# Inputs of the recurrent blocks as two half-partition DMAs on two queues, with other edits around the loop (one Trainium2 core)

## The chip, the core and the metric

The program runs on one core of one Trainium2 chip. The metric is device microseconds of one execution, lower is better. In the traces PE is TensorE's matmuls, PEld its weight loads, DVE VectorE, ACT ScalarE, POOL GpSimd, SP the engine whose queue issues DMAs; SPq is the issue of a DMA on it. "L375" is line 375 of the program that is named.

## The reference, cut to what matters

A gated linear recurrence per head (4 batches, 8 heads, 768 steps, 40 features), then a soft mixture of experts on its output, then a product of two projections:

```
for t in range(768):                                  # per batch and head
    m_new = max(f[t] + m, i[t]); C = exp(f+m-m_new)*C + exp(i-m_new)*outer(v, k); n likewise with k
    y[t] = sigmoid(o_gate[t]) * (C @ q) / max(|n @ q|, 1)
x = y as (3072, 320)
logits = x @ phi; d = softmax over tokens; slots = d.T @ x
slot_out = relu(slots @ w1[e]) @ w2[e]                # 8 experts, 4 slots each
x = softmax(logits over slots) @ slot_out
out = (x @ w_a) * (x @ w_b) @ w_out
```

## The kernel before

Engines are programmed one by one, each with an instruction list written out by hand, and meet only through semaphores (`wait_ge`, `then_inc`). The work before the experts is the recurrence in chunked form. The 32 heads are 8 units (u) of 4 heads, and a unit's 768 steps are 3 blocks of 4 chunks of 64 steps: 24 blocks n = 0 to 23, u = n // 3.

**Start.** DVE scans the gates and makes G (running log decay) and b (log input weight less G), each 32x768. Both are cut into three bf16 parts that sum to the f32 value, side by side in the tile `PT`: G's by ACT (casts) and POOL (subtracts, L469), b's by DVE alone (L655 to L658, cast and subtract in turn). SP writes the parts to DRAM (`scratch_b`, `scratch_G`) and `load_exponents(u)` reads each unit's rows back into `LE` and `RE`, the operands of the exponent matmuls. DVE then makes `dm`, from which PE makes the chunk decays, and PE runs 16 transposes that nobody reads (`keep_clock`) before block 0.

**Loop.** In iteration n PE runs `updates(n)`, `exponents(n + 1)`, `scores(n + 1)`, `inner(n)`, `carried(n)` and, from n = 6, `turn(n - 6)`: four transposes (L1026) of finished output, which ACT copies out of PSUM (L545). ACT takes the exponential of `exponents(n)` (L555), POOL scales block n's k by its last column (L491, semaphore `ks_sb`), DVE multiplies scores and exponentials (L684), steps the state (L701) and sums the two output parts (`gather`, L713 and L714); after each unit come a denominator, POOL's product with it (`gate`) and the product with the recurrence's output (`x_out`, L727). The sigmoids of the output gates are ACT's, one batch at a time (L531); the last batch's stands between the exponentials of blocks 1 and 2.

**Loads.** `load_block(n)` on SP is five DMAs: one of k in two layouts on 128 partitions (L375, `kkb`, three buffers), two of q on 40 partitions each (L380) and two of v on 64 each (L386; four buffers each). It waits until the buffer's last readers are done. Behind blocks 8 and 14 SP issues one expert weight tile each (L427, 128x5120 floats), and after the loop two more (L433).

**End.** The last unit isn't finished as a whole: `x_last(n)` on DVE (L735 to L741) finishes blocks 21, 22 and 23 each by itself. `turn(17)` ends iteration 23; `turn(18)` to `turn(23)` follow, through three PSUM banks, all copied by ACT. Then come the logits (first matmuls `ps<-xTreg,small`), the experts and the output tiles, which the change doesn't touch except for the form of two weight loads.

Of the kernel before, what the change touches and what calls it, by code (L numbers as in the profile page):

```python
# [36 lines left out]
ALU = mybir.AluOpType  # L37
# [10 lines left out]
L = 64  # L48
NC = S // L
NCP = NC // 2  # L50
HU = 4
# [58 lines left out]
def build(nc, qT, kk, v1, og, ig, fg, phi, w1, w2, wab, wo, cst, out):  # L110
    with ExitStack() as ctx:
# [63 lines left out]
        qb = [view(take(4 * CB * L), 4 * CB * L).rearrange("r (p h t) -> r p h t", p=2, h=2) for _ in range(NQ)]  # L175

        KF, KT = 2 * CB * L, 2 * HU * D
        kkb = [view(take(KF + KT), KF + KT) for _ in range(3)]
        kb = [x[:, 0:KF].rearrange("r (p t) -> r p t", p=2) for x in kkb]
        knb = [x[:, KF:KF + KT].rearrange("r (c h e) -> r c h e", c=2, h=HU) for x in kkb]  # L180
        VB = 2 * HU * VW + 8
        vb = [view(take(2 * VB), 2 * VB).rearrange("r (a n) -> r a n", a=2) for _ in range(NQ)]
# [3 lines left out]
        Wb = [view(take(512), 512).rearrange("r (c h t) -> r c h t", c=2, h=HU) for _ in range(2)]  # L186
# [10 lines left out]
        def gview(i, n):  # L197
# [65 lines left out]
        ld_k = [sem(f"ld_k{i}") for i in range(3)]  # L263
        ld_q = [sem(f"ld_q{i}") for i in range(NQ)]
        ld_v = [sem(f"ld_v{i}") for i in range(NQ)]
# [98 lines left out]
        def _(sp):  # L364
# [4 lines left out]
            def load_block(n):  # L369
                u, blk = n // NBLK, n % NBLK  # L370
                t0, tn = blk * CB * L, CB * L
                if n >= 3:
                    sp.wait_ge(s_ps, n - 2)
                    sp.wait_ge(ks_sb, n - 2)
                sp.dma_start(kkb[n % 3], kk[u, blk]).then_inc(ld_k[n % 3], 16)  # L375
                if n >= NQ:
                    sp.wait_ge(x_ps, n - NQ + 1)
                for hp in range(2):
                    rows = slice(64 * hp, 64 * hp + D)
                    sp.dma_start(qb[n % NQ][rows, :, hp, :], qT[u, hp, :, :, t0:t0 + tn]).then_inc(ld_q[n % NQ], 16)  # L380
                if n >= NQ:
                    sp.wait_ge(u_ps, n - NQ + 1)
                    sp.wait_ge(y_ps, n - NQ + 1)
                for par in range(2):

                    sp.dma_start(vb[n % NQ][64 * par:64 * par + 64, par, 0:2 * HU * VW],  # L386
                                 v1[u, 64 * par:64 * par + 64, blk, :]).then_inc(ld_v[n % NQ], 16)

            def load_exponents(u):
# [3 lines left out]
                if u == 0:  # L393
                    sp.wait_ge(rows_done, 1)
                    sp.wait_ge(b_out, 16)
                elif u == 1:
                    sp.wait_ge(rows_done_1, 1)
                sp.dma_start(LE[r][L:L + 3 * HU, :], scr_b[u * HU:(u + 1) * HU].rearrange("h k s -> (h k) s")).then_inc(ld_exp[r], 16)
                if u == 0:
                    sp.wait_ge(G_out, 16)  # L400
                for par in range(2):
                    rows = slice(L + R_B + 3 * par, L + R_B + 3 * par + 3)
                    src = scr_G[:, u * HU:(u + 1) * HU].rearrange("k h (c a t) -> k h c a t", a=2, t=L)
                    sp.dma_start(RE[r][rows], src[:, :, :, par, :]).then_inc(ld_exp[r], 16)  # L404

            for b in range(B - 1):
                sp.dma_start(xtok[:, b], og[b]).then_inc(ld_og[b], 16)
            sp.wait_ge(zeroed, 4)
            load_block(0)
# [12 lines left out]
            for n in range(4, NB):
# [3 lines left out]
                if n in (8, 14):  # L426
                    sp.dma_start(w1s[n // 12], w1[n // 12]).then_inc(ld_w1p[n // 12], 16)  # L427
# [4 lines left out]
            for i in (2, 3):  # L432
                sp.dma_start(w1s[i], w1[i]).then_inc(ld_w1p[i], 16)  # L433
# [21 lines left out]
        def _(pool):  # L455
# [11 lines left out]
            for k in range(2):  # L467
                pool.wait_ge(cut_done, k + 1)
# [55 lines left out]
        def _(act):  # L524
# [14 lines left out]
            for b in range(B - 1):  # L539
                sigmoid(b)  # L540
# [772 lines left out]
```

## Time and profile before

| | |
|---|---|
| median of 3 runs | 290.74 us (290.41 to 292.62) |
| profiled execution, its own time | 292.25 us |
| its span, first to last instruction | 290.2 us |
| mean granted TensorE clock | 0.965 of full |
| busy: PE, PEld, DVE, ACT, POOL | 250.7, 208.8, 181.8, 88.3, 61.8 us |
| loop (block 0's exponents to the end of `turn(17)`) | 23.0 to 142.9 us |
| first logits | 147.35 us |

Rows are from the profiled execution, in us from the span's start. A timeline row is: start, duration, engine, line, operation, output<-input, shapes, count, and in brackets how long the engine had been idle before it and who ended that.

### The profile page before, as it was taken

The numbers are of one execution on the slowest core, as the hardware profiler recorded it, in microseconds if no ns is written. First come the engines' busy times: TensorE is split into PE (matmuls) and PEld (weight loads), VectorE is DVE, ScalarE is ACT, GpSimd is POOL, SyncE is SP. The second block draws the span as 40 slices with busy tenths as digits, with TensorE's granted clock in tenths as the row PEclk, the third lists the DMA queues.
The fourth block names the chain that finished last, engine by engine and source line by source line (L and its number), as shares of the span: only waits on it lengthen the run. The fifth ranks groups of instructions, "written<-read, shape, count | busy, mean of one in ns | idle before, by whom it ended". The sixth has DMA issues, their size and how long they took to land.

```text
span 290.2 us, 7910 instructions
## 1 busy us (share of the span) xinstructions
PE 250.7 (86%) x3264; PEld 208.8 (72%) x3264; DVE 181.8 (63%) x462; ACT 88.3 (30%) x145; POOL 61.8 (21%) x92
## 2 busy tenths in 40 slices
PE   0557698855999499999799998999799999999996
PEld 0546687845999499899657935556656668999995
DVE  6963667842787277888916823355886867555550
ACT  3683511210222113222236002343800003444441
POOL 9502152311325123427030321331000000000000
PEclk9999999995899779999999999999979999999999
DMA  7827866689658965660299999990000000322222
GB/s 247 351 52 252 221 189 196 183 370 262 179 149 323 288 190 153 184 203 2 78 420 419 424 416 381 436 399 24 2 0 0 0 2 0 113 93 90 80 82 90
DMA packets 20131, 54.73 MB, mean 189 GB/s; under 512 B 3744, under 2 KB 14144, under 8 KB 18432
## 3 DMA queue, kind: packets, MB, share of 16 engines
q1 hardware_dynamic: 20096, 54.23, 54.1%
q8 instruction: 26, 0.43, 0.6%
q14 instruction: 9, 0.07, 0.1%
HBM read 49.99 MB, written 4.23 MB: 187 GB/s over the span
## 4 chain that ended last, share of the span: by engine, by line
PE 60%; SPq 12%; DVE 11%; DMA 11%; issue 2%; ACT 2%; DVEq 0%
PE ps L935 52%; DMA attn<-kk 8%; SPq L380 5%; SPq L386 4%; PE ps L1148 3%; PE ps L1026 2%; DVE attn L701 1%; SPq L375 1%; ACT xTreg L545 1%; DMA attn<-scratch_G 1%; DMA scratch_G<-xTreg 1%; PE ps L1154 1%; DMA xTreg<-ig 1%; SPq L404 1%; DVE attn L684 1%
## 5 line engine op out<-in xcount | busy, mean ns | idle before, releaser
L935 PE MATMUL ps<-attn 128*64 128x41 f32 (+3 forms) x2016 | 92.4, 253 | 17.9 <-DMA attn<-kk 10.4
L935 PEld LDWEIGHTS ps<-attn 128*64 128x64 f32 (+1 forms) x2016 | 86.7, 141 | 25.1 <-DMA attn<-kk 10.9
L491 POOL TENSOR_TENSOR attn<-attn 128x160 f32<-128x160 f32 x48 | 21.1, 461 | 86.2 <-issue 54.4
L701 DVE SCALAR_TENSOR_TENSOR attn<-attn,small,ps 128x41 f32<-128x41 f32 x176 | 31.0, 249 | 5.0 <-PE ps L935 5.0
L545 ACT COPY xTreg<-ps 128x512 f32<-128x512 f32 x24 | 13.6, 593 | 63.8 <-PE ps L1026 63.8
L935 PE MATMUL ps<-woreg,tlow 128*128 128x320 f32 x96 | 28.0, 454 | 2.5 <-DVE tlow L885 2.5
L935 PE MATMUL ps<-Whr,Phr 128*128 128x320 f32 x96 | 30.0, 313 | 0.0
L935 PE MATMUL ps<-Whr,Plr 128*128 128x320 f32 x96 | 29.7, 309 | 0.0
L935 PE MATMUL ps<-Wlr,Phr 128*128 128x320 f32 x96 | 29.6, 309 | 0.0
L684 DVE TENSOR_TENSOR attn<-ps,attn 128x512 f32<-128x512 f32 x24 | 16.5, 688 | 19.6 <-issue 13.6
L935 PEld LDWEIGHTS ps<-woreg,tlow 128*128 128x128 f32 x96 | 18.4, 200 | 11.8 <-DVE tlow L885 4.6
L555 ACT ACTIVATE attn<-ps 128x512 f32<-128x512 f32 x24 | 14.3, 597 | 27.3 <-PE ps L935 27.3
L904 DVE TENSOR_TENSOR Plr<-tail,Phr 128x512 fp32r<-128x512 f32 x20 | 13.8, 691 | 13.0 <-ACT Phr L610 13.0
L713 DVE TENSOR_TENSOR attn<-ps,small 128x328 f32<-128x328 f32 x24 | 12.0, 498 | 14.1 <-PE ps L935 14.1
L935 PEld LDWEIGHTS ps<-Whr,Phr 128*128 128x128 f32 x96 | 18.0, 188 | 0.6 <-issue 0.5
L935 PEld LDWEIGHTS ps<-Wlr,Phr 128*128 128x128 f32 x96 | 18.0, 188 | 0.1
L935 PEld LDWEIGHTS ps<-Whr,Plr 128*128 128x128 f32 x96 | 18.0, 188 | 0.0
L587 ACT COPY tail<-ps 128x512 f32<-128x512 f32 x20 | 10.8, 589 | 18.5 <-PE ps L1148 18.5
L318 POOL TENSOR_TENSOR freg<-small 128x512 f32<-128x512 f32 x6 | 8.6, 1429 | 34.6 <-PE ps L1148 22.0
L318 DVE TENSOR_TENSOR freg<-small 128x512 f32<-128x512 f32 x18 | 12.5, 718 | 5.4 <-PE ps L1148 5.4
L1026 PE MATMUL ps<-small,xreg 128*80 128x128 f32 x96 | 14.9, 287 | 0.8 <-ACT xTreg L545 0.8
L610 ACT CAST Phr<-tail 128x512 fp32r<-128x512 f32 x20 | 12.1, 620 | 10.7 <-PE ps L935 10.7
(158 smaller groups left out, 339.8 us busy)
## 6 DMA issues: line engine op xcount, KB each, us to landing
attn<-kk SPq DMA_DIRECT2D x24, 416.0 KB, 4.5
front<-w SPq DMA_DIRECT2D x2, 2560.0 KB, 10.6
tail<-w SPq DMA_DIRECT2D x2, 2560.0 KB, 12.1
xTreg<-w SPq DMA_DIRECT2D x4, 1280.0 KB, 12.9
attn<-v SPq DMA_DIRECT2D x48, 82.0 KB, 3.2
xreg<-og SPq DMA_DIRECT2D x4, 960.0 KB, 7.0
attn<-qT SPq DMA_DIRECT2D x48, 80.0 KB
xreg<-w SPq DMA_DIRECT2D x3, 1280.0 KB, 10.9
```

The source lines that it names most:

```text
L318: return eng.tensor_tensor(Pt[t % 4], fixed(Ed[:, t], 16), shifted(Ed[:, t], 0, 16), ALU.mult)
L380: sp.dma_start(qb[n % NQ][rows, :, hp, :], qT[u, hp, :, :, t0:t0 + tn]).then_inc(ld_q[n % NQ], 16)
L491: last = g.tensor_tensor(ksb[n % 2][:, c, 0:HU * D].rearrange("r (h e) -> r h e", h=HU), knb[n % 3][:, c], last_col[:, c].unsqueeze(2).to_ ...
L545: s.copy(xT[:, u % 2, u // 2, CB * blk:CB * blk + CB].rearrange("r c t -> r (c t)"), turn_ps(m)[:, :]).then_inc(xT_sb, 1)
L555: s.activation(Eb[n % 2], psE[n % 2][:], ACT.Exp).then_inc(e_sb, 1)
L610: s.copy(Ph[t % 3], Pm[t]).then_inc(one["ph_sb"], 1)
L684: v.tensor_tensor(Wb[n % 2].rearrange("r c h t -> r (c h t)"), psS[n % 2][:], Eb[n % 2], ALU.mult).then_inc(w_sb, 1)
L701: last = v.scalar_tensor_tensor(out=C[:, cc + 1, p], in0=C[:, cc, p], scalar=dcy[:, 2 * u + p, cc:cc + 1], in1=pUv[:, p, c, 0:VW], op0=ALU ...
L713: chain(v.tensor_tensor(T, pXv[:, :, :, 0:VW], eg.unsqueeze(3).to_broadcast([128, 2, CB, VW]), ALU.mult))
L904: v.tensor_tensor(Pl[t % 3], Pm[t], Ph[t % 3].bitcast(F32), ALU.subtract).then_inc(one["pl_sb"], 1)
L935: return t_.matmul(o_, l_, r_, start=start, stop=stop)
L1026: last = t_.transpose(turn_ps(m)[0:80, 128 * c:128 * c + 128], xtok[:, u // 2, blk * CB + c, 80 * (u % 2):80 * (u % 2) + 80], ident)
```

## The change

1. **Blocks by halves.** q, v and k of a block lie in one DRAM array and one tile `in_b` (four buffers, 2512 columns). Partitions 0 to 63 take columns 0 to 1671, partitions 64 to 127 columns 840 to 2511; q is padded from 40 to 64 rows. SP loads the lower half, ACT's queue the upper one (`load_upper`; in the loop after the exponential of block n - 2). All of a block's readers wait for both halves, and both wait for all readers of the buffer four blocks ago.
2. **Parts of b** by four two-input subtracts; the casts are gone (L710 to L714 of the program after).
3. **First unit's operands** go from `PT` to `LE` and `RE` straight, by 10 small DMAs; the DRAM copies serve units 1 to 7. G's parts are stored with the even and the odd chunks apart, so a read of them is 768 bytes in a row (128 before).
4. **Gates** by tanh: sigmoid(x) = 0.5 tanh(x/2) + 0.5, two ACT instructions for half a batch, spread over the loop. The list that is built has one table load for all of ACT's start and loop; before it had five.
5. **Weights in pieces.** w1's first two tiles come as 10 pieces of 128x1024 behind blocks 4 to 15, except 6 and 12, where a batch of gates is loaded; the last two tiles as 10 pieces after the loop.
6. **End.** DVE keeps the denominators (`den_last`) and block 23's products; POOL takes those of 21 and 22. `turn(17)` stands ahead of `carried(23)`; DVE copies `turn(21)` and `turn(23)` out of PSUM, ACT the rest.
7. DVE's product of scores and exponentials goes to another tile (`Ed`'s place in `small`).

```diff
+        in_b = [view(take(HALF + OTHER), HALF + OTHER) for _ in range(NQ)]
+        qb = [two(x, 0, [[CB * L, 2], [HALF + VF, 2], [1, CB * L]]) for x in in_b]
+        vb = [two(x, QF, [[VF + KF + KT, 2], [1, VF + 8]]) for x in in_b]
@@ SP
             def load_block(n):
-                sp.dma_start(kkb[n % 3], kk[u, blk]).then_inc(ld_k[n % 3], 16)
-                for hp in range(2):
-                    sp.dma_start(qb[n % NQ][rows, :, hp, :], qT[u, hp, :, :, t0:t0 + tn]).then_inc(ld_q[n % NQ], 16)
-                for par in range(2):
-                    sp.dma_start(vb[n % NQ][64 * par:64 * par + 64, par, 0:2 * HU * VW],
-                                 v1[u, 64 * par:64 * par + 64, blk, :]).then_inc(ld_v[n % NQ], 16)
+                if n >= NQ:
+                    done = n - NQ + 1
+                    sp.wait_ge(s_ps, done)
+                    sp.wait_ge(ks_sb, done)
+                    sp.wait_ge(u_ps, done)
+                    sp.wait_ge(y_ps, done)
+                    sp.wait_ge(x_ps, done)
+                else:
+                    sp.wait_ge(zeroed, n + 1)
+                sp.dma_start(in_b[n % NQ][0:64, 0:HALF], blk_in[u, blk, 0]).then_inc(ld_b[n % NQ], 16)
...
             sp.wait_ge(parts_b, 1)
+            for h in range(HU):
+                sp.dma_start(LE[0][L + 3 * h:L + 3 * h + 3, :], PT[h:h + 1, :, S:2 * S]).then_inc(ld_exp[0], 16)
+            sp.wait_ge(parts_G, 1)
+            for par in range(2):
+                for k in range(3):
+                    row = L + R_B + 3 * par + k
+                    sp.dma_start(RE[0][row:row + 1].rearrange("r h c t -> r h (c t)"), PT[0:HU, k, 384 * par:384 * par + 384]).then_inc(ld_exp[0], 16)
...
-                if n in (8, 14):
-                    sp.dma_start(w1s[n // 12], w1[n // 12]).then_inc(ld_w1p[n // 12], 16)
+                if n in (6, 12):
+                    sp.dma_start(xtok[:, n // 6 + 1], og[n // 6 + 1]).then_inc(ld_og[n // 6 + 1], 16)
+                elif 4 <= n < 16:
+                    j = n - 4 - (n > 6) - (n > 12)
+                    cols = slice(j % 5 * F, j % 5 * F + F)
+                    sp.dma_start(w1s[j // 5][:, cols], w1[j // 5, :, cols]).then_inc(ld_w1p[j // 5], 16)
@@ ACT
+            for n in range(3):
+                load_upper(n)
             act.wait_ge(ld_const, 16)
...
+            def sigmoid(u):
+                act.wait_ge(ld_og[u // 2], 16)
+                x = xtok[:, u // 2, :, 80 * (u % 2):80 * (u % 2) + 80]
+                s.activation(x, x, ACT.Tanh, scale=0.5).then_inc(tanh_done, 1)
+                act.wait_ge(tanh_done, u + 1)
+                s.activation(x, x, ACT.Copy, scale=0.5, bias=0.5).then_inc(sig_done, 1)
...
             for n in range(NB):
-                if n == 2:
-                    sigmoid(B - 1)
...
                 s.activation(Eb[n % 2], psE[n % 2][:], ACT.Exp).then_inc(e_sb, 1)
+                if 2 <= n < NB - 2:
+                    load_upper(n + 2)
+                if n >= 4 and n % NBLK == 1 and n // NBLK + 1 < NU:
+                    sigmoid(n // NBLK + 1)
                 if n >= 7:
                     xT_evac(n - 7)
@@ DVE
             chain(v.tensor_tensor(b_, t2_g, GB[:, 0:S], ALU.subtract))
-            chain(v.tensor_copy(PT[:, 0, S:2 * S], b_))
+            chain(v.tensor_tensor(PT[:, 0, S:2 * S], t2_g, GB[:, 0:S], ALU.subtract))
             chain(v.tensor_tensor(R, b_, PT[:, 0, S:2 * S], ALU.subtract))
-            chain(v.tensor_copy(PT[:, 1, S:2 * S], R))
+            chain(v.tensor_tensor(PT[:, 1, S:2 * S], b_, PT[:, 0, S:2 * S], ALU.subtract))
@@ PE
                 inner(n)
+                if n == NB - 1:
+                    turn(n - 6)
                 carried(n)
```

The order at three places. **First place, SP's queue from the load of block 8 to that of block 9** (`kk`, `qT`, `v`: the five DMAs of a block; `w`: expert weights). Before:

```order
L375 DMA attn<-kk 128x832 [waits ks_sb,s_ps]
L380 DMA attn<-qT 40x2x256 [waits x_ps]
L380 DMA attn<-qT 40x2x256
L386 DMA attn<-v 64x328 [waits y_ps,u_ps]
L386 DMA attn<-v 64x328
L427 DMA front<-w 128x5120
L375 DMA attn<-kk 128x832 [waits ks_sb,s_ps]
```

After, from behind block 6 to behind block 8 (`blk_in`: a block's lower half; `og`: gates):

```order
L444 DMA xreg<-og 128x1920
L404 DMA attn<-blk_in 64x1672 [waits y_ps,u_ps,x_ps,ks_sb,s_ps]
L414 DMA attn<-scratch_b 12x768 [waits e_ps]
L418 DMA attn<-scratch_G 3x4x384 x2
L448 DMA front<-w 128x1024
L404 DMA attn<-blk_in 64x1672 [waits y_ps,u_ps,x_ps,ks_sb,s_ps]
L448 DMA front<-w 128x1024
```

Between two blocks stands now at most a fifth of a weight tile, or a batch of gates.

**Second place, the start.** ACT before, from its first row to G's second part:

```order
L334 ACT_TABLE_LOAD
L334 CAST attn<-small 82x768 [waits ld_const]
L337 CAST attn<-small 76x384 x4
L535 CAST xTreg<-xTreg 32x768 [waits G_done]
L536 ACTIVATE xTreg<-xTreg 32x768
L538 CAST xTreg<-xTreg 32x768 [waits R_done]
```

ACT after, the same stretch (`zeroed`: POOL has cleared the buffer):

```order
L574 DMA attn<-blk_in 64x1672 [waits zeroed] x3
L339 ACT_TABLE_LOAD
L339 CAST attn<-small 82x768 [waits ld_const]
L342 CAST attn<-small 76x384 x4
L590 CAST xTreg<-xTreg 32x6x2x64 [waits G_done]
L591 ACTIVATE xTreg<-xTreg 32x768
L593 CAST xTreg<-xTreg 32x6x2x64 [waits R_done]
L574 DMA attn<-blk_in 64x1672 [waits zeroed]
```

Three half loads, which wait for POOL's clears, stand now ahead of ACT's table load and of all that it does for G.

**Third place, DVE's end of the loop**, from the scores of block 23 to its own products. Before:

```order
L684 TENSOR_TENSOR attn<-ps,attn 128x512 [waits y_ps,s_ps,e_sb]
L735 SCALAR_TENSOR_TENSOR attn<-attn 128x2x4 [waits t_sb]
L736 TENSOR_SCALAR attn<-attn 128x2x4 [waits dve]
L738 TENSOR_TENSOR xreg<-xreg,attn 128x2x4x40 [waits sig_done,dve]
L740 RECIPROCAL attn<-attn 128x2x4
L741 TENSOR_TENSOR xreg<-xreg,attn 128x2x4x40 [waits dve]
L713 TENSOR_TENSOR attn<-ps,small 128x2x164 [waits x_ps,y_ps]
L714 TENSOR_TENSOR attn<-attn,ps 128x2x164 [waits dve]
```

After, the same stretch:

```order
L740 TENSOR_TENSOR small<-ps,attn 128x512 [waits y_ps,s_ps,e_sb]
L789 SCALAR_TENSOR_TENSOR attn<-attn 128x2x4 [waits t_sb]
L790 TENSOR_SCALAR attn<-attn 128x2x4 [waits dve]
L791 RECIPROCAL attn<-attn 128x2x4 [waits dve]
L769 TENSOR_TENSOR attn<-ps,small 128x2x164 [waits x_ps,y_ps]
L770 TENSOR_TENSOR attn<-attn,ps 128x2x164 [waits dve]
```

The two products of block 21 are gone from DVE's list ahead of block 22's `gather`; those of block 22 are gone in the same way ahead of block 23's.

## Rows read from the trace of the kernel before

**Rows 1.** The page, the chain that ended last, by engine.

```profile
PE 60%; SPq 12%; DVE 11%; DMA 11%; issue 2%; ACT 2%; DVEq 0%
```

**Rows 2.** Timeline of PE, turns and what stands between them.

```profile
55.98 0.63 PE L1026 MATMUL ps<-small,xreg 128*80 128x128 f32 x4
...
60.04 0.64 PE L1026 MATMUL ps<-small,xreg 128*80 128x128 f32 x4
...
68.42 4.92 PE L935 MATMUL ps<-attn 128*64 128x128 f32 x64 [6.71 <-DMA attn<-kk]
73.27 1.04 PE L1026 MATMUL ps<-small,xreg 128*80 128x128 f32 x4
...
94.35 0.63 PE L1026 MATMUL ps<-small,xreg 128*80 128x128 f32 x4
...
104.55 0.77 PE L1026 MATMUL ps<-small,xreg 128*80 128x128 f32 x4
```

**Rows 3.** Windows: busy us (instructions) by engine, then clock, DMA share, GB/s.

```profile
117.04:129.59 12.55, 12.39 (x267) 11.48 (x265) 10.31 (x36) 3.55 (x6) 4.54 (x8) 1.00 0.71 196
170.00:190.00 20.00, 19.12 (x196) 10.31 (x186) 6.58 (x11) 6.25 (x12) 4.88 (x3) 1.00 1.00 414
```

**Rows 4.** The chain in order of time, 55 to 70 us: start, us, what.

```profile
56.96 11.42 DMA attn<-kk
```

**Rows 5.** DMA issues by line, ns min/median/max, and landings.

```profile
L386 SPq DMA_DIRECT2D attn<-v x48: 529/590/1762, 9.0 to 128.3; - x48
...
DMA to landing us min/median/max: 2.3/3.2/9.6
```

**Rows 6.** DMA in 104 to 131 us: packets, MB, share of 16 engines.

```profile
q1 hardware_dynamic: 3173, 4.59, 60.6%
...
attn<-kk SPq DMA_DIRECT2D x5, 416.0 KB, 3.8
```

**Rows 7.** Timeline of the start, DVE and POOL.

```profile
9.79 0.94 DVE L654 TENSOR_TENSOR xTreg<-xTreg 32x768 f32<-32x768 f32 x1
9.92 2.31 POOL L469 TENSOR_TENSOR xTreg<-xTreg 32x768 f32<-32x768 f32 x1 [2.80 <-ACT xTreg L535]
10.77 1.88 DVE L655 CAST xTreg<-xTreg 32x768 bf16<-32x768 f32 x1
...
13.17 1.95 POOL L469 TENSOR_TENSOR xTreg<-xTreg 32x768 bf16<-32x768 f32 x1 [0.94 <-ACT xTreg L538]
13.66 1.88 DVE L657 CAST xTreg<-xTreg 32x768 bf16<-32x768 f32 x1
15.57 0.94 DVE L658 TENSOR_TENSOR xTreg<-xTreg 32x768 bf16<-32x768 f32 x1
16.45 0.54 DVE L334 CAST attn<-small 82x768 bf16<-82x768 f32 x1
```

**Rows 8.** Timeline, a POOL and a DVE product of the experts' stage.

```profile
196.64 1.15 POOL L318 TENSOR_TENSOR freg<-small 128x512 f32<-128x512 f32 x1 [5.03 <-PE ps L1148]
...
197.03 1.31 DVE L318 TENSOR_TENSOR freg<-small 128x512 f32<-128x512 f32 x1 [0.50 <-PE ps L1148]
```

**Rows 9.** Timeline of PE and ACT, first iterations.

```profile
19.45 3.65 PE L1032 MATMUL ps<-small 128*128 128x128 f32 x16
...
25.20 2.43 PE L935 MATMUL ps<-attn 128*64 128x128 f32 x48 [0.67 <-DMA attn<-qT]
...
29.51 1.80 ACT L531 ACTIVATE xreg<-xreg 128x1920 f32<-128x1920 f32 x1 [3.03 <-DMA xreg<-og]
...
32.00 3.36 PE L935 MATMUL ps<-attn 128*64 128x128 f32 x80 [1.47 <-issue]
...
36.20 1.07 PE L935 MATMUL ps<-attn 82*64 82x256 bf16 x16 [0.85 <-DMA attn<-scratch_G]
```

**Rows 10.** Timeline of ACT and PE, end of the loop.

```profile
144.26 3.04 ACT L545 COPY xTreg<-ps 128x512 f32<-128x512 f32 x6 [0.79 <-PE ps L1026]
...
147.35 3.11 PE L935 MATMUL ps<-xTreg,small 128*32 128x384 f32 x36
```

More of the change, by code:

```diff
@@ L107, in constants, with build @@
     return c
-def build(nc, qT, kk, v1, og, ig, fg, phi, w1, w2, wab, wo, cst, out):
+def build(nc, blk_in, og, ig, fg, phi, w1, w2, wab, wo, cst, out):
     with ExitStack() as ctx:
@@ L185, in build @@
               for _ in range(2)]
-        Wb = [view(take(512), 512).rearrange("r (c h t) -> r c h t", c=2, h=HU) for _ in range(2)]
+        Wb = [Ed[:, 8 * i:8 * i + 8].rearrange("r (c h) t -> r c h t", c=2) for i in range(2)]
         Eb = [view(take(512), 512) for _ in range(2)]
@@ L262, in build @@
         ld_w2e = [sem(f"ld_w2e{i}") for i in range(E)]
-        ld_k = [sem(f"ld_k{i}") for i in range(3)]
-        ld_q = [sem(f"ld_q{i}") for i in range(NQ)]
-        ld_v = [sem(f"ld_v{i}") for i in range(NQ)]
+        ld_b = [sem(f"ld_b{i}") for i in range(NQ)]
         ld_exp = [sem(f"ld_exp{i}") for i in range(2)]
@@ L401, in load_exponents @@
                 for par in range(2):
                     rows = slice(L + R_B + 3 * par, L + R_B + 3 * par + 3)
[L403 to L409, printed above, removed]
-            sp.wait_ge(parts_b, 1)
+                    src = scr_G[:, u * HU:(u + 1) * HU].rearrange("k h (a s) -> k h a s", a=2)
@@ L432, in _ @@
             for i in (2, 3):
-                sp.dma_start(w1s[i], w1[i]).then_inc(ld_w1p[i], 16)
+                for j in range(5):
+                    cols = slice(j * F, j * F + F)
+                    sp.dma_start(w1s[i][:, cols], w1[i, :, cols]).then_inc(ld_w1p[i], 16)
             sp.wait_ge(one["logits_ps"], 2)
@@ L465, in _ @@
             pool.wait_ge(C_zero, 2)
-            for k in range(2):
-                pool.wait_ge(cut_done, k + 1)
-                left = g.tensor_tensor([GR, PT[:, 2]][k][:, 0:S], [GB, GR][k][:, 0:S], PT[:, k, 0:S], ALU.subtract)
-                left.then_inc([R_done, parts_G][k], 1)
+            pool.wait_ge(cut_done, 1)
+            g.tensor_tensor(by_par(GR[:, 0:S]), by_par(GB[:, 0:S]), halves(0), ALU.subtract).then_inc(R_done, 1)
+            pool.wait_ge(cut_done, 2)
+            g.tensor_tensor(halves(2), by_par(GR[:, 0:S]), halves(1), ALU.subtract).then_inc(parts_G, 1)
             pool.wait_ge(parts_G, 1)
@@ L503, in _ @@
                         last.then_inc(x_sb, 1)
+            for i in range(2):
+                T, d, x = last_unit(NB - NBLK + i)
+                pool.wait_ge(den_done, NU + i)
+                pool.wait_ge(sig_done, NU)
+                for p in range(2):
+                    last = g.tensor_tensor(x[:, p], x[:, p], T[:, p, :, 0:D], ALU.mult)
+                last.then_inc(last_half, 1)
+                pool.wait_ge(last_half, i + 1)
+                for p in range(2):
+                    last = g.tensor_tensor(x[:, p], x[:, p], d[:, 1, p].unsqueeze(2).to_broadcast([128, CB, D]), ALU.mult)
+                last.then_inc(last_sb, 1)
             pool.wait_ge(y_ps, NB)
@@ L756, in _ @@
             gather(NB - 1)
+            den_last(NB - 1)
             x_last(NB - 1)
+            for m in (NB - 3, NB - 1):
+                v_.wait_ge(t_ps, m + 1)
+                v.tensor_copy(turned(m), turn_ps(m)[:, :]).then_inc(xT_sv, 1)
             v.memset(ones, 1.0)
```

155 lines of the change are left out of this document (81 added, 74 removed).

## The prediction

> **What bounds the kernel now.** I read the chain that ended last first: 60% of it is PE, but 12% is SP's issuing and 11% DMA [rows 1], so PE isn't bound by its own work everywhere. The timeline of PE shows where. One `turn` ends each iteration of the loop, so the distance of two turns is an iteration. At 55.98 and 60.04 they are 4.06 us apart; the next is at 73.27, because PE stood idle for 6.71 us for k of the next block and then ran 64 matmuls in 4.92 us [rows 2]. The chain names the transfer: k was issued at 56.96 and took 11.42 us, as it was queued behind the 2.6 MB weight tile [rows 4]. The same again between 94.35 and 104.55 [rows 2]. Undisturbed, three iterations take 12.55 us with PE busy in 12.39 of them [rows 3]: 4.18 each, PE-bound, and no edit touches PE's work there. After the loop the experts' stage is PE's (19.12 of 20 us busy, while the DMA engines run full at 414 GB/s [rows 3]), and the change leaves its order alone. So there are four places to cost: the two stalls, the transfers that replace them, the start, and the end of the loop.
>
> **The two stalls.** They cost 73.27 - 60.04 - 4.06 = 9.17 and 104.55 - 94.35 - 4.06 = 6.14 us, 15.3 in all, the slow matmuls behind them included [rows 2]. In pieces, a block waits for at most 0.52 MB (1.27 us at 414 GB/s) or a batch of gates of 0.98 MB (2.37 us), where an undisturbed k took 3.8 us from issue to landing [rows 6]. **-15.3**, if nothing else in the DMA queue is late next.
>
> **What is late next: the DMA engines.** A block is now 128 x 1672 x 4 bytes = 0.856 MB (0.758 before). What rate do half-partition transfers reach? In 104 to 131 us, where only blocks were loaded, 4.59 MB took 60.6% of 27 us: 281 GB/s per busy time [rows 6]. That is a mix. The five k transfers (2.13 MB, 128 partitions) at 414 would take 5.1 of the 16.4 busy us; the other 2.46 MB, all on 64 partitions or fewer, then ran at 2.46 / 11.3 = 217. So the bounds are 217 and 414 GB/s. I take 281: half a partition range, but long rows (6.7 KB), and two queues whose halves can lie over each other.
> The time that is available, from the load of block 4 (0.6 us into iteration 1) to `scores(15)` (1.0 into iteration 14): five iterations without a turn at 3.8 (below), eight at 4.18, and 0.4 more, less 2.0 for landing (2.3 at least for an 82 KB transfer [rows 5], 0.3 of it its bytes) = 50.8 us. Needed: 12 blocks x 3.05 = 36.6, 9 pieces x 1.27 = 11.4, 2 batches of gates x 2.37 = 4.7, together 52.7. Short by 1.9; I add 1.2 because a load can't run further ahead than four buffers, so that the two batches come as bursts. **+3.1** as short waits in iterations 6 to 13. At 414 GB/s it is 0, at 217 it is 12 x 3.94 + 16.1 - 50.8 + 1.2 = 13.8. From block 16 on 3.05 is under 4.18 and hidden. A load's wait for all readers of the buffer adds nothing: before, q and v waited for the same block, and the operands and the piece that stand behind it on SP are due iterations later.
>
> **ACT's new work.** An upper half's issue is not in the trace; SP's for 64 partitions takes 0.59 us [rows 5]. ACT is busy for 3.55 / 3 = 1.18 us of an iteration [rows 3]; with the issue 1.8, and with the tanh and the copy (half of 1.80 each [rows 9]) 3.6 in every third one. The next exponential is due 3.8 to 4.2 us after the last, so this is hidden; `load_upper`'s waits (block n - 2 done) have passed before the exponential of block n can start. It would cost once an issue took over 1 us.
>
> **The start** has three terms.
> *Parts of b, +0.9.* Before, two casts of 1.88 and two subtracts of 0.94 ended at 16.51 [rows 7]. But a wider cast takes 0.54 [rows 7]: the two ended 0.4 us after POOL's subtracts did (12.23 and 15.12), and POOL's own first one (9.92) lay over DVE's subtract to 10.73. Each waits for the other, and a DVE product with two SBUF inputs does so too: 1.31 us for 128x512 when a POOL product ran until 197.79 [rows 8]. Replacing the casts therefore doesn't save 2 x 0.94. Four subtracts end at 10.77 + 4 x 0.98 = 14.7 if POOL never holds them; with both of POOL's (12.23 - 10.73 = 1.5 each) in between, at 17.7. ACT's part comes later as well: three half loads wait for POOL's clears ahead of it. I take 17.2, that is +0.7. Block 0's exponents follow 6.5 us behind by PE (decays and the 16 transposes of 3.65 us up to 23.1 [rows 9]), or by SP: ten issues of 0.3 to 0.6 and a landing of 2.3 or more, 5.3 to 8.5 us. Say +0.9 in all; ends -1.8 and +3.
> *First iterations, -3.0.* PE's waits for q (0.67), for q and k behind the gates' batch (1.47) and for unit 1's operands (0.85) go [rows 9]: blocks 0 to 2 are loaded long before, and with the tanh there is no table load or sigmoid (29.51 [rows 9]) between the exponentials of blocks 1 and 2. Unit 1's operands are issued at about 26 and due at 33.
> *Iterations 2 to 6, -1.6.* From 36.20 [rows 9] to 55.98 [rows 2] is 19.8 us. An iteration without a turn needs 4.18 less the turn's 0.6 on PE, and DVE some more: 3.8 (3.6 at the least). From the exponents to an iteration's end is 3.0, so 3.0 + 4 x 3.8 = 18.2. SP's five issues per block become one.
> Together **-3.7** (ends -7 and 0).
>
> **The end, -1.3.** Two pairs of products (0.49 us each) leave DVE ahead of the last two `gather`s, which PE and then everything wait for. After it ACT copied six turns in 3.04 us, right up to the logits [rows 10]; now DVE takes two, and `turn(17)` fills an idle stretch of PE. DVE's chain then ends about 1 us earlier and the last copies 0.3 sooner behind it; 0 if POOL, which takes those products in four operations of 0.45 us, is late.
>
> **The sum.** -15.3 + 3.1 - 3.7 - 1.3 = -17.2 us. Against the profiled execution's own 292.25 this is 275.0; that execution lay 1.5 above the median of the runs, so against 290.74 it is **273.5 us**. The experts' stage moves as a whole: its weights are asked for at the loop's end as before, and ten issues of 0.6 us instead of two stay behind transfers of 1.27.
>
> **Rivals.** *Fast transfers.* The two halves overlap fully, 320 GB/s or more: no short waits, 270.4; with parts of b that POOL doesn't hold (-2.5), 267.9. For it: rows of 6.7 KB. Chance 0.18.
> *The halves take turns.* Transfers to partitions 0 to 63 and 64 to 127 run one after the other at half width, 217 GB/s as above [rows 6]: +13.8 instead of +3.1, 284.2. For it: that rate is what the half-wide transfers of this trace give. Against it: those were short and shared one queue. Chance 0.12.
> By the Trainium skill, page "SBUF — State Buffer", section "Can I just issue two DMAs to hit both halves?", two such DMAs side by side ran only 6% faster than one, and its table has 196 GB/s for one of 1 MiB on partitions 0 to 63. By that rule a block takes 0.856 / 208 = 4.1 us and the kernel about 286, an estimate; this trace, which has no pair of long halves, shows neither.
> *Slower than before.* The same mechanism with a lower rate. The whole gain of 20.3 us (without transfers' cost) is gone when 12 t + 16.1 - 50.8 + 1.2 + 8 (t - 4.18) = 20.3, t being a block's transfer: t = 4.35 us, 197 GB/s. At 180 GB/s t is 4.76 and the kernel takes 298.6: PE would wait for `blk_in` in every iteration to the last. Against it: no stretch of block loads in the trace is that slow per busy time. Chance 0.04.
>
> **How the numbers follow.** The likeliest, 0.66: 270 to 278. The range 268 to 282 leaves out most of the turn-taking rival and the slower one, and some of the fastest. A measurement of this kernel tells changes over about 1% from none. Faster by over 1%, under 287.8: all but the slower case and a little of the turn-taking one, 0.94; within 1% 0.03; slower 0.03.
>
> **What the profile after will show.** Turns 4.1 to 4.5 us apart with no idle of several us and a granted clock of 1.00 throughout; short PE waits for `blk_in` in iterations 6 to 13, and 0.9 DMA share there; DVE's subtract chain with one or two of 1.5 to 2.5 us and an end near 17; block 0's exponents near 24; `turn(17)` near 124; logits about 17 us earlier than 147.35. It is wrong if the turns drift to 5 us (rate of halves), if ACT's issues take over 1 us, or if the start lies 3 us off.

## The result, and the profile after

The changed kernel takes **302.71 us** (median of 4 runs, 302.33 to 304.38), the kernel before beside it 290.69 (290.41 to 292.62): 1.041 times as long, 95% interval 1.035 to 1.047. The forecast was 273.5, with 282 as its upper end. The profiled execution has a span of 300.7 us against 290.2. The profiled execution of the kernel before took 292.25 us, 1.5 more than its median, so a difference between traces comes out that much more favourable to a change. Some kernels below have executions that took over 1.5% longer than their fastest one; where a reading hangs on them, all times are given.

The chain that ended last now names the blocks' loads. Before, issues of SP held 12% of it and DMA 11% [rows 1]; now SP's issuing is 2%, and DMA 18%, nearly all of it one tensor:

```profile
PE 62%; DMA 18%; DVE 12%; issue 3%; SPq 2%; ACT 1%; ACTq 0%; DVEq 0%
PE ps L997 53%; DMA attn<-blk_in 17%; PE ps L1212 3%; PE ps L1087 2%; DVE attn L757 2%; SPq L432 1%; SPq L427 1%; DVE xTreg L713 1%; DVE xTreg L711 1%; PE ps L1093 1%; PE ps L1218 1%; DMA xTreg<-ig 1%; DVE attn L769 1%; ACT freg L622 1%; DV
```

PE's timeline has lost the two big stalls of [rows 2], and has gained many smaller ones. The first turn comes at 63.62 instead of 55.98, the next ones lie 5.5 to 8.1 us apart, and only from 121.34 on is the distance 4.06 again:

```profile
63.62 0.78 PE L1087 MATMUL ps<-small,xreg 128*80 128x128 f32 x4
...
67.58 1.98 PE L997 MATMUL ps<-attn 128*64 128x128 f32 x16 [2.14 <-DMA attn<-blk_in]
...
71.71 0.63 PE L1087 MATMUL ps<-small,xreg 128*80 128x128 f32 x4
...
77.90 1.08 PE L1087 MATMUL ps<-small,xreg 128*80 128x128 f32 x4
...
121.34 0.63 PE L1087 MATMUL ps<-small,xreg 128*80 128x128 f32 x4
125.40 0.63 PE L1087 MATMUL ps<-small,xreg 128*80 128x128 f32 x4
```

The windows say why (busy us by engine, then granted clock, DMA share, GB/s). Over 90 us the DMA engines are fully busy and move 227 to 249 GB/s. The experts' stage, again at share 1.0, moves 420 (414 in [rows 3]). So a share of 1.0 isn't a rate; the two columns have to be read together. PE's clock is granted at 0.83 on the mean of 45 to 75 us, a mixture of its two levels (1.2 and 2.4 GHz); PE stands idle for 7.8 of these 30 us, nearly all of it in waits for blocks:

```profile
30.00:45.00 15.00, 12.65 (x304) 11.73 (x302) 11.80 (x45) 4.40 (x6) 4.53 (x8) 1.00 1.00 249
45.00:75.00 30.00, 22.20 (x386) 20.75 (x388) 13.95 (x46) 5.57 (x8) 6.25 (x12) 0.83 1.02 227
75.00:120.00 45.00, 32.81 (x636) 28.68 (x631) 26.09 (x86) 14.31 (x20) 11.55 (x21) 0.96 1.02 234
...
162.00:182.00 20.00, 19.34 (x216) 15.09 (x212) 12.95 (x33) 5.22 (x10) 3.81 (x2) 1.00 1.02 420
```

The DMA view of the same 90 us (30 to 120) has the queues (q1 is SP's, q10 ACT's: packets, MB, share of the 16 engines' time) and what was queued: count, size, and median time from issue to landing. A half takes some 12 us to land (5 where only blocks are loaded); pieces and gates, which are 128 partitions wide, are later still:

```profile
q1 hardware_dynamic: 3455, 14.70, 72.0%
q10 hardware_dynamic: 1148, 6.16, 28.8%
...
attn<-blk_in SPq DMA_DIRECT2D x15, 418.0 KB, 11.9
attn<-blk_in ACTq DMA_DIRECT2D x15, 418.0 KB, 12.6
front<-w SPq DMA_DIRECT2D x10, 512.0 KB, 17.5
xreg<-og SPq DMA_DIRECT2D x2, 960.0 KB, 18.1
```

In 121 to 146 us only blocks are loaded, as in the window of [rows 6]: (2.29 + 2.19) MB in 74.1% of 25 us is 242 GB/s per busy time.

```profile
q10 hardware_dynamic: 432, 2.29, 38.2%
q1 hardware_dynamic: 459, 2.19, 35.9%
```

At the start, each of DVE's rounding subtracts ends 0.8 us after POOL's beside it (13.06 and 12.24, 16.35 and 15.54), which is nearly the 0.94 us that one takes undisturbed: it seems to start its work only when POOL's has ended. Below are DVE and POOL, then SP's issues of the ten small transfers, then PE:

```profile
10.44 1.80 POOL L491 TENSOR_TENSOR xTreg<-xTreg 32x768 f32<-32x768 f32 x1 [3.42 <-ACT xTreg L590]
10.79 2.27 DVE L711 TENSOR_TENSOR xTreg<-xTreg 32x768 bf16<-32x768 f32 x1
...
13.19 2.35 POOL L493 TENSOR_TENSOR xTreg<-xTreg 32x768 bf16<-32x768 f32 x1 [0.94 <-ACT xTreg L593]
14.07 2.28 DVE L713 TENSOR_TENSOR xTreg<-xTreg 32x768 bf16<-32x768 f32 x1
16.39 0.94 DVE L714 TENSOR_TENSOR xTreg<-xTreg 32x768 bf16<-32x768 f32 x1
```

```profile
17.43 2.96 SPq L427 DMA_DIRECT2D attn<-xTreg  x4
20.43 3.74 SPq L432 DMA_DIRECT2D attn<-xTreg  x6
```

```profile
25.28 3.04 PE L997 MATMUL ps<-attn 82*64 82x256 bf16 x56 [1.74 <-DMA attn<-xTreg]
```

### The profile page after: what moved, and what is told of

It is laid out like the page before. It is cut to its first block, busy times and chain, and to the rows that moved or that the text cites. A ratio compares the mean times of both kernels' runs of the same rounds, so it can differ in the third digit from the quotient of the medians.

```text
span 300.7 us, 7912 instructions
## 1 busy us (share of the span) xinstructions
PE 252.1 (84%) x3264; PEld 209.4 (70%) x3264; DVE 183.2 (61%) x460; ACT 91.2 (30%) x151; POOL 65.2 (22%) x100
## 3 DMA queue, kind: packets, MB, share of 16 engines
q10 hardware_dynamic: 1920, 10.27, 14.2%
## 4 chain that ended last, share of the span: by engine, by line
PE 62%; DMA 18%; DVE 12%; issue 3%; SPq 2%; ACT 1%; ACTq 0%; DVEq 0%
PE ps L997 53%; DMA attn<-blk_in 17%; PE ps L1212 3%; PE ps L1087 2%; DVE attn L757 2%; SPq L432 1%; SPq L427 1%; DVE xTreg L713 1%; DVE xTreg L711 1%; PE ps L1093 1%; PE ps L1218 1%; DMA xTreg<-ig 1%; DVE attn L769 1%; ACT freg L622 1%; DVE tlow L384 1%
## 5 line engine op out<-in xcount | busy, mean ns | idle before, releaser
L997 PE MATMUL ps<-attn 128*64 128x41 f32 (+3 forms) x1632 | 80.5, 255 | 26.1 <-DMA attn<-blk_in 17.2
L997 PEld LDWEIGHTS ps<-attn 128*64 128x64 f32 (+1 forms) x1632 | 70.6, 142 | 34.5 <-DMA attn<-blk_in 19.9
L514 POOL TENSOR_TENSOR attn<-attn 128x160 f32<-128x160 f32 x48 | 21.1, 460 | 98.2 <-DMA attn<-blk_in 46.7
L740 DVE TENSOR_TENSOR small<-ps,attn 128x512 f32<-128x512 f32 x24 | 16.6, 691 | 23.4 <-issue 16.5
L600 ACT COPY xTreg<-ps 128x512 f32<-128x512 f32 x22 | 12.7, 587 | 57.2 <-PE ps L1087 57.2
L997 PE MATMUL ps<-woreg,tlow 128*128 128x320 f32 x96 | 26.8, 437 | 2.7 <-DVE tlow L947 2.7
L997 PEld LDWEIGHTS ps<-woreg,tlow 128*128 128x128 f32 x96 | 17.4, 190 | 11.9 <-DVE tlow L947 5.3
L997 PE MATMUL ps<-attn,small 128*64 128x96 f32 x384 | 22.3, 259 | 0.0
L997 PEld LDWEIGHTS ps<-attn,small 128*64 128x64 f32 x384 | 19.8, 145 | 0.2
```

Source lines behind the costliest of these rows:

```text
L514: last = g.tensor_tensor(ksb[n % 2][:, c, 0:HU * D].rearrange("r (h e) -> r h e", h=HU), knb[n % NQ][:, c], last_col[:, c].unsqueeze(2).to ...
L600: s.copy(turned(m), turn_ps(m)[:, :]).then_inc(xT_sb, 1)
L740: v.tensor_tensor(Wb[n % 2].rearrange("r c h t -> r (c h t)"), psS[n % 2][:], Eb[n % 2], ALU.mult).then_inc(w_sb, 1)
L997: return t_.matmul(o_, l_, r_, start=start, stop=stop)
```

## The experiments

I ran twelve kernels in three groups, each group against the kernel before on the same chip: 289.81 us (288.81 to 291.73) for e1 to e4, 289.27 (287.88 to 291.19) for e5 to e8, 289.98 (288.76 to 291.37) for e9 to e12. A ratio is to that; intervals are of 95%. The first group was run when only the trace above was known: the halves, the two queues, the pieces and the total of bytes were all suspects.

**e1, both halves in one queue.**

```diff
+                sp.dma_start(in_b[n % NQ][64:128, OTHER:OTHER + HALF], blk_in[u, blk, 1])...
-                s.dma_start(in_b[n % NQ][64:128, OTHER:OTHER + HALF], ...)   # ACT's, in load_upper
```

> The kernel after, with both halves of a block issued on SP, one behind the other (ACT issues none). Three theories of why the loop's DMA engines moved only 234 GB/s. Half width: a transfer into 64 partitions reaches about half the rate wherever it is issued: stays slow, 298 to 308 us, 200 to 240 GB/s at a share of 1.0 in the loop. Two queues: the two queues' packets disturb each other and one queue would not: 276 to 285 us. Bytes: the rate belongs to the mix of reads and no form helps: 300 to 305 us.

Measured: 309.40 us, ratio 1.068 (1.061 to 1.075), just over the 298 to 308 of the half-width theory. The four runs are 305.30, 308.04, 310.76 and 310.94; even the fastest is above the changed kernel's slowest, 304.38. Its window 45 to 75, at the same share as above:

```profile
45.00:75.00 30.00, 20.33 (x406) 18.32 (x404) 15.95 (x55) 6.15 (x10) 7.36 (x14) 0.93 1.02 232
```

One queue isn't better than two: by the two faster runs it is 1 to 2% worse, by the median 2.6%. So two queues were not what slowed the kernel. By the Trainium skill, page "SBUF — State Buffer", section "Can I just issue two DMAs to hit both halves?", two such transfers side by side gain only 6% over one; the traces agree in kind (from 30 to 120 us the loop moves 234 GB/s with two queues and 230 with one).

**e2, whole blocks of full width.** The host writes the zeros that the two halves leave out, so a block is one transfer of 128 x 2512 numbers: 1.286 MB instead of 0.856.

```diff
-                sp.dma_start(in_b[n % NQ][0:64, 0:HALF], blk_in[u, blk, 0])...
+                sp.dma_start(in_b[n % NQ], blk_in[u, blk])...
-                s.dma_start(in_b[n % NQ][64:128, OTHER:OTHER + HALF], ...)   # ACT's
```

> The kernel after, each block as ONE transfer of the whole tile, 128 partitions x 2512 columns (1.286 MB, zeros included, 50% more bytes) on SP. Half width: 1.286 / 414 = 3.1 us per block instead of about 3.8, the loop needs 12 x 3.1 + 16.1 = 53 us for 51 available, so stalls of at most 5 us in all: 275 to 283 us. Two queues: the same, as there is one queue. Bytes: 234 GB/s stays, 5.5 us per block: over 320 us.

Measured: **280.74 us**, ratio 0.969 (0.963 to 0.975). With half as many bytes again per block, the kernel takes 22 us less than the changed one. Window 45 to 75:

```profile
45.00:75.00 30.00, 27.31 (x584) 24.53 (x582) 22.86 (x77) 10.16 (x15) 9.80 (x18) 1.00 1.01 412
```

The same engines at the same share move 412 GB/s where the halves move 227. PE waits for `blk_in` for 1.7 us in all instead of 17.2.

**e3, k at full width, q and v by halves.** 128 x 832 in one transfer, and 64 x 840 in each queue.

```diff
+                sp.dma_start(in_b[n % NQ][:, OTHER:HALF], kk_in[u, blk])...
+                sp.dma_start(in_b[n % NQ][0:64, 0:OTHER], blk_in[u, blk, 0])...
+                s.dma_start(in_b[n % NQ][64:128, HALF:HALF + OTHER], blk_in[..., 1])...
```

> The kernel after, k of a block as one 128-partition transfer of 832 columns on SP, q and v as two halves of 64 x 840, on SP and ACT as before. Bytes as in the kernel after. Half width: 0.43 MB at 414 and 0.43 at about 235, 2.9 us per block: 276 to 286 us. Two queues: both queues still at work, so 290 to 303 us. Bytes: 300 to 305 us.

Measured: 291.78 us, ratio 1.005 (1.001 to 1.009), between e2 and the changed kernel at the changed kernel's bytes. Half of a block's bytes at full width give 269 GB/s in 45 to 75 us, at share 1.04. This is a miss: the half-width theory had said 276 to 286, and 290 to 303 was what disturbance between two queues would give. By itself e3 speaks for the queues; e6 below decides against them.

**e4, the pieces alone, in the kernel before.**

```diff
-                if n in (8, 14):
-                    sp.dma_start(w1s[n // 12], w1[n // 12])...
+                if 4 <= n < 16 and n not in (6, 12):
+                    sp.dma_start(w1s[j // 5][:, cols], w1[j // 5, :, cols])...
```

> The kernel before with one edit alone: the first two weight tiles in ten pieces of 128x1024 behind blocks 4 to 15 (not 6 and 12). Blocks keep their five transfers. If the price of the change is in the block transfers, the two stalls of 9.2 and 6.1 us go and little comes in their place: 275 to 280 us. If the pieces themselves (their 4 KB rows among the blocks) are what slowed the loop: 290 to 300 us.

Measured: 283.86 us, ratio 0.979 (0.974 to 0.983), less of a gain than expected. From the first turn to the logits it takes 78.6 us instead of 91.4, so most of the two stalls is gone. But the first turn comes at 61.53 instead of 55.98: in iterations 3 to 6 PE now stands idle, 3.03 us at one place. The row gives that wait no releaser, but the chain that ended last names k of block 6: SP issues it at 45.24, right behind a piece (44.56), and it lands 6.46 us later, where an undisturbed k takes 3.8 [rows 6]. POOL waits 4.71 us for it, and PE goes on 1.33 us after it has landed. How much of the 6.46 is the piece's is not separated.

```profile
53.03 6.66 PE L937 MATMUL ps<-attn 128*64 128x128 f32 x116 [3.03 <-issue]
```

e2 differs from the changed kernel in width, row length, bytes and ACT's issues all at once. The second group takes them apart. In e5 and e6 half of the partitions don't get the columns that the computation needs, so the two stand for the time alone.

**e5, the same bytes at full width.** Each block one transfer of 128 x 1672.

```diff
-                sp.dma_start(in_b[n % NQ], blk_in[u, blk])...              # e2
+                sp.dma_start(in_b[n % NQ][:, 0:HALF], blk_in[u, blk])...
```

> The changed kernel with every block loaded by one transfer of 128 partitions x 1672 numbers on SP's queue: the 0.856 MB of the two halves, at full width (e2 moved 1.286 MB a block). The columns of q, v and k then stand wrong for partitions 64 to 127 and the last 840 columns stay as cleared, so this run computes other numbers; its instructions and times are otherwise those of the changed kernel. Theory A (half the partitions make the rate): the blocks run at 400 GB/s or more, 2.1 us each, no wait of PE for a block after iteration 2, 272 to 279 us, at or some us below e2's 280.7. Theory B (the row length of 6.7 KB, and its mixture with pieces of 1.3 to 4 KB rows, makes the rate): 235 GB/s as in the changed kernel, about 300 us.

Measured: **276.15 us**, ratio 0.954 (0.947 to 0.961). Bytes, row length (6.7 KB) and pieces are those of the changed kernel; only the width isn't, and there is one queue. Beside e1, which has one queue too, a block is one transfer of 128 x 1672 instead of two of 64 x 1672: 276.15 us against 309.40. The DMA view of 30 to 120 us, against the one above:

```profile
q1 hardware_dynamic: 5216, 25.55, 78.0%
...
attn<-blk_in SPq DMA_DIRECT2D x20, 836.0 KB, 6.5
front<-w SPq DMA_DIRECT2D x10, 512.0 KB, 7.5
xreg<-og SPq DMA_DIRECT2D x2, 960.0 KB, 9.2
```

That is 25.55 / (0.78 x 90) = 364 GB/s per busy time, less than the 400 that I had expected, and 20.86 / (1.008 x 90) = 230 with the halves. Theory B (row length and mixture) falls.

**e6, the same at full width, by two queues.** Two transfers of 128 x 836, SP's and ACT's.

```diff
+                sp.dma_start(in_b[n % NQ][:, 0:HALF // 2], blk_in[u, blk, 0])...
+                s.dma_start(in_b[n % NQ][:, HALF // 2:HALF], blk_in[..., 1])...   # load_upper
```

> As e5, with the 1672 numbers of each of 128 partitions in two transfers of 836, one on SP's queue and one on ACT's: both queues and ACT's issues as in the changed kernel, the same bytes, full width. It leaves the same part of the computation wrong as e5. Theory A (half width): as e5, 272 to 279 us. Theory C (two queues at once, or ACT's issues in its row): most of the loss is still there, 290 us or more. Shorter rows (3.3 KB) may cost a little: up to 3 us above e5 under theory A.

Measured: **275.09 us**, ratio 0.950 (0.943 to 0.957). It issues from the same engines at the same places as the changed kernel, with the same bytes, at the same semaphores. Theory C falls too. Its window 45 to 75, and its turns, which are undisturbed from first to last (only three of the rows stand here):

```profile
45.00:75.00 30.00, 28.39 (x625) 26.23 (x621) 24.20 (x83) 11.02 (x16) 10.25 (x19) 1.00 0.99 363
```

```profile
55.09 0.63 PE L1087 MATMUL ps<-small,xreg 128*80 128x128 f32 x4
59.15 0.63 PE L1087 MATMUL ps<-small,xreg 128*80 128x128 f32 x4
...
121.88 0.63 PE L1087 MATMUL ps<-small,xreg 128*80 128x128 f32 x4
```

**e7, e2 with the pieces later.**

```diff
-                elif 4 <= n < 16:
+                elif n in (8, 9, 10, 13, 14, 16, 17, 18, 20, 21):
```

> e2 (whole blocks of 1.286 MB at full width) with the ten pieces of w1's first two tiles behind blocks 8, 9, 10, 13, 14, 16, 17, 18, 20 and 21 instead of 4 to 15. If in e2 the DMA engines were what PE waited for in iterations 2 to 10 (their share was near 1 there, PE waits for blocks 1.7 us), this takes 2 to 4 us off: 277 to 279. If they weren't, it is e2's 280.7.

Measured: 279.58 us, ratio 0.965 (0.959 to 0.970). The interval overlaps e2's, so by the times it is unclear. In the traces the way from the first turn to the logits is 134.29 - 56.66 = 77.6 us against 136.19 - 55.62 = 80.6: 3 us shorter, as expected; but the matmuls at the start take 1.5 us longer in this trace (see e9).

**e8, the changed kernel with whole weight tiles.**

```diff
-                elif 4 <= n < 16:
-                    sp.dma_start(w1s[j // 5][:, cols], w1[j // 5, :, cols])...
+                if n in (8, 14):
+                    sp.dma_start(w1s[n // 12], w1[n // 12])...
```

> The changed kernel with w1's first two tiles whole again, behind blocks 8 and 14: only the splitting of the weights is undone. If the loop of the changed kernel is bound by the total of its transfers at some 235 GB/s, as I now think, splitting them hardly matters: 299 to 306 us, the waits gathered at two places of 8 to 12 us. If the pieces themselves are slow or in the blocks' way, this is faster, under 297. If pieces save what I forecast (two stalls of 15.3 us in all), it is slower, 313 or more.

Measured: 302.02 us (296.10, 301.80, 302.23 and 306.79; they spread too far for a ratio), beside the changed kernel's 302.71. This rules out that the pieces save 15 us here, for that needed 313 or more. It doesn't decide between "hardly matters" (299 to 306) and "faster" (under 297), as the fastest run lies in the latter. In the trace, of the slowest run, the lost time is gathered at four places where turns lie 8.9 to 11.5 us apart, and 30 to 120 us move 228 GB/s, as the changed kernel's 234. That fits a loop bound by the total of its transfers, but does not show it.

The third group asks for the small terms, on e7.

**e9, the first unit's operands through memory again.**

```diff
-            for h in range(HU):
-                sp.dma_start(LE[0][...], PT[h:h + 1, :, S:2 * S])...
-            for par in range(2):
-                for k in range(3):
-                    sp.dma_start(RE[0][row:row + 1]..., PT[0:HU, k, ...])...
             sp.dma_start(scr_b, ...); sp.dma_start(scr_G, ...)
+            load_exponents(0)
```

> e7 (whole blocks at full width, pieces later) with the first unit's operands by way of device memory again, as the kernel before has them (three loads in place of ten, behind the two stores). In e7 the ten small transfers keep SP for 6.7 us and PE waits 1.3 us for the last one. Expected: block 0's exponents at 24.0 instead of 25.3, by PE's own transposes, and 1 to 1.5 us less in all: about 278. If the detour through memory costs the 2 us of landing that it was made to save, they stay at 25 or later and the time at 279.6.

Measured: **275.62 us**, ratio 0.950 (0.945 to 0.955), 4 us better than e7 (of the group before) where 1 to 1.5 were expected. PE's rows of e7, of e11 and of e9, in this order:

```profile
25.35 4.56 PE L992 MATMUL ps<-attn 82*64 82x256 bf16 x56 [1.34 <-DMA attn<-xTreg]
```

```profile
25.28 3.05 PE L990 MATMUL ps<-attn 82*64 82x256 bf16 x56 [1.34 <-DMA attn<-xTreg]
```

```profile
23.74 3.08 PE L987 MATMUL ps<-attn 82*64 82x256 bf16 x56
```

The exponents start at 23.74 with no wait, 1.6 us earlier. Another 1.5 us are of a kind that I hadn't expected: the matmuls behind the wait took 4.45 to 5.8 us in the traces of e1, e3, e5, e7, e8 and e10, and 3.05 in those of the changed kernel, e2, e6 and e11, behind the same wait. Without it (e9, e12) they took 3.04 and 3.08. In e9 the detour begins at 17.24 with a store and its last load is issued by 21.1; in e7 the last of the ten direct transfers is issued at 24.2. Of the lead, 3.0 us stand at the exponential of block 4 and 2.3 are left at the logits. Another 1.2 us lie behind them, in the part that the edit doesn't touch; that part takes 141.8 to 143.1 us in the fourteen traces, with no order that an edit explains. So the traces give the direct transfers a price of 2.3 to 3.0 us; for the rest of the 4 they show no cause.

**e10, the casts back.**

```diff
-            chain(v.tensor_tensor(PT[:, 0, S:2 * S], t2_g, GB[:, 0:S], ALU.subtract))
+            chain(v.tensor_copy(PT[:, 0, S:2 * S], b_))
```

and the same for the second part.

> e7 with the two casts back in place of the subtracts that round parts of b. Expected: DVE's chain ends at 16.5 instead of 17.4, the exponents 0.8 us earlier at 24.5, the time about 279, within what a measurement can tell. If the differences save what two casts of 1.88 against two subtracts of 0.94 would (1.9 us), they end at 19 or later and the run is slower by 1.5.

Measured: 279.51 us, ratio 0.963 (0.959 to 0.967): no difference from e7 that the times can show. In the trace parts of b end 1 us sooner and block 0's exponential starts at 24.99 instead of 26.02. At the first turn 0.8 us of it are left, at the logits none (134.34 against 134.29). A cast waits for POOL as the subtract does, but takes 1.88 us there and the subtract 2.28:

```profile
10.63 1.88 DVE L706 CAST xTreg<-xTreg 32x768 bf16<-32x768 f32 x1
...
13.53 1.88 DVE L708 CAST xTreg<-xTreg 32x768 bf16<-32x768 f32 x1
```

**e11, the gates by a sigmoid.**

```diff
-                s.activation(x, x, ACT.Tanh, scale=0.5)...
-                s.activation(x, x, ACT.Copy, scale=0.5, bias=0.5)...
+                s.activation(x, x, ACT.Sigmoid)...
```

> e7 with the gates by one sigmoid in place of a tanh and a copy, still one unit at a time. I forecast that the tanh takes a table load (1.3 us) from between the exponentials and makes iterations 0 to 2 shorter. Expected: a table load before and after each of the eight gates' functions, 2.6 us of ACT each time, two of them before block 0's exponentials (hidden) and six in the loop; ACT is idle for 2.5 us of an iteration, so each costs PE at most 1 us: 280 to 285. If ACT's slack takes them all, 279.6.

Measured: 278.39 us, ratio 0.960 (0.956 to 0.964); the interval overlaps e7's, and the sigmoid is in no case slower. ACT's slack takes both table loads of each unit (ACT's timeline of e11):

```profile
39.54 0.60 ACT L602 ACTIVATE attn<-ps 128x512 f32<-128x512 f32 x1 [3.34 <-PE ps L990]
40.15 1.28 ACT L583 ACT_TABLE_LOAD   x1
41.45 1.00 ACT L583 ACTIVATE xreg<-xreg 128x960 f32<-128x960 f32 x1
42.47 1.28 ACT L602 ACT_TABLE_LOAD   x1
43.83 0.60 ACT L602 ACTIVATE attn<-ps 128x512 f32<-128x512 f32 x1
```

From `turn(0)` to `turn(17)` both e11 and e7 take 71.5 us. The tanh brought nothing, and the 280 to 285 that I had expected without it were too dear.

**e12, e9 and e10 together**: whole blocks at full width, pieces behind later blocks, casts, operands through memory.

> e7 with both the casts and the way through device memory back: e9 and e10 together. Expected: exponents of block 0 at 23.1 as in the kernel before, 2.2 us earlier than in e7, and 277.4 us. If the rest of the loop is bound by its transfers, which start no earlier, less of it arrives: 278.5.

Measured: **274.55 us**, ratio 0.948 (0.943 to 0.953), exponents at 22.51. It is 2.9 us better than expected. By the median this is the fastest of those that do the whole computation, though its interval overlaps e9's: 15.4 us below the kernel before, some 28 below the changed one.

## Why the prediction was wrong

The stretches of the loop, in us of the profiled executions. Exp(n) is ACT's exponential of block n; the forecast is the sum of the prediction's terms for that stretch. By the medians the changed kernel is 12.0 us slower and e6 14.2 faster, where these traces have 10.5 and 17.0: the trace of the kernel before is of an execution of 292.25 us, 1.5 above the median beside the changed kernel and 3.0 above the one beside e6.

| stretch | before | forecast | after | e6 |
|---|---|---|---|---|
| start to Exp(0) | 23.49 | +0.9 | +2.2 | +2.2 |
| Exp(0) to Exp(4) | 16.53 | -3.0 | -3.3 | -2.9 |
| Exp(4) to `turn(0)` | 15.96 | -1.6 | +8.7 | -0.3 |
| `turn(0)` to `turn(16)` | 82.11 | -15.3 + 3.1 | +4.8 | -15.3 |
| `turn(16)` to logits | 9.26 | -1.3 | -0.9 | -0.9 |
| logits to the end | 142.85 | 0 | -1.0 | +0.2 |
| sum | 290.2 | -17.2 | +10.5 | -17.0 |

**The step that failed is "What is late next": "I take 281: half a partition range, but long rows (6.7 KB), and two queues whose halves can lie over each other", with the pieces and gates costed at 414 beside it.** The blocks alone run at 242 GB/s, nearer to the lower bound of 217 than to 281, and the second queue is worth 1 to 2.6% of the time (e1), not a rate between the two bounds. The larger error is the other half of the sum: pieces (512 KB) and gates (960 KB) were costed as if they ran by themselves. They are 128 partitions wide, but share the engines with the halves, and the whole loop moves 230 GB/s. The 17.0 MB of my sum (12 x 0.856 + 9 x 0.524 + 2 x 0.983) then need 74 us of the 50.8, short by 23 and not by 1.9. Of these 21 us more, 6 are the blocks' own rate (12 x 0.856 at 242 instead of 281) and 15 come from the company that they keep. Measured against e6, which has the same bytes at full width, the term was 8.9 + 20.1 = 29 us instead of 3.1. The windows from the exponential of block 4 to `turn(16)` take it apart: both kernels run 1724 matmuls there, the changed one in 88.1 busy us of 111.5 at a mean clock of 0.94, e6 in 79.8 of 82.5 at 1.00. So 20.7 us are idle time of PE and 8.3 are matmuls that ran slower behind the waits, a cost for which the sum had no term. The sign that the prediction had named for this, turns that drift to 5 us, is what the trace shows: 5.5 to 8.1.

**The rivals.** "The halves take turns" was nearest to the mechanism (that width sets the rate is shown, that the two halves literally alternate is not) and "Slower than before" the outcome, with a threshold set too low, at 197 GB/s for the block (196 when its sum is worked out again). That threshold came from a sum with 16.1 us for pieces and gates. With all 17.0 MB at one rate r, the whole gain of 20.3 us is gone when 17.0 / r = 50.8 - 1.2 + 20.3 = 69.9 us, that is at 243 GB/s; the trace's 230 lies just under it. Such a rate was inside the bounds that I had given for the blocks (217 to 414), so with everything in the queue at the blocks' rate "slower" would have been near even, and not a chance of 0.04.

**The two stalls**, -15.3: right, had nothing else been late. In e6 the stretch that held them is 15.3 us shorter, and in e4 the pieces alone give back 12.8 between first turn and logits.

**ACT's new work**: right that it is hidden. An issue takes 0.47 us, and e6, with all of ACT's issues, has turns 4.06 apart. But what I credited the tanh with, in -3.0 for the first iterations, was not its doing: the size was right (-3.3), and e11, without the tanh, has most of it (-2.7). The sigmoid of before waited 3.03 us for its gates there [rows 9], and those now come earlier and elsewhere.

**The start**: +2.2 instead of +0.9. Parts of b took +0.8, where I had said +0.7; the rest is SP, whose ten issues take 0.62 to 0.74 us each (6.7 us in all) where I had 0.3 to 0.6. Their operands land 7.9 us after parts of b, inside the 5.3 to 8.5 that I gave for SP's way, while my +0.9 went by PE's 6.5; so PE waits for 1.3 to 1.7 us. e9 shows the price: the ten direct transfers cost more than they save.

**Iterations 2 to 6**, -1.6: even undisturbed (e6) only -0.3. A mis-sized term: in e6 the distance of two exponentials is 3.7 to 3.8 us, as I took it, from block 2 to 4 and from 5 to 6, but 4.3 from 4 to 5 and 4.4 from 6 to 7. The kernel before takes as long there (4.4 and 4.5), and in both DVE has a unit's denominator or its product with the output (1.15 us) to do. I had 3.8 for each iteration; that DVE's work sets the difference is likely, but not shown.

**The end**, -1.3: -0.9, right in kind. **The experts' stage**: -1.0, inside what the traces of all kernels spread over there (141.8 to 143.1 us).

## What to carry to other kernels

Give a transfer all 128 partitions, even where that means storing and loading zeros: here blocks with 50% more bytes made the kernel 22 us faster. When a narrow transfer is to share the engines with others, cost the whole queue at the narrow one's rate, as here it slowed what ran beside it too; and read DMA share and GB/s together, since a full share says nothing of the rate. A detour by memory in five transfers (two stores, three loads) can be shorter than a direct way in ten, as each of these issues held its queue for 0.6 us and more.

## What the runs showed that I had not expected

Transfers of half the partitions hold the rate of full-width ones beside them: 230 GB/s for a mixture in which about a third of the bytes (10 pieces of 0.524 MB and 2 batches of gates of 0.983 MB among the 20.86 MB of 30 to 120 us) are 128 partitions wide, against 364 with all of it at full width. If each kind had kept its own rate, the 13.7 MB of halves at 242 and the 7.2 MB at 414 would have kept the engines busy for 74 us; they were busy for 91. The mixture of e3, with k at full width too, still reached only 269. Why a narrow transfer slows a wide one is open.

A wait of 1.3 to 1.7 us of PE at the start was followed, in six traces of ten, by matmuls that took a third to a half longer (the first eight a mean of 421 ns in e7 and 279 in e11, the next 32, of 128x64 by 128x128, 371 and 272), while the granted clock of these windows reads 1.00 in both. What decides between the two is open.
